# Attention with a top-32 mask and two expert layers on one core: the first five slots written out, the hidden product turned earlier, and the last 64 keys of two heads turned together

## The reference

```python
# attention, for each batch and head
scores = q @ k.T / sqrt(64)
kth    = 32nd largest score of each row
scores = where(scores >= kth, scores, -1e9)
attn   = exp(scores - max);  attn /= attn.sum() + 1e-9
x      = attn @ v                     # heads side by side: 1152 x 512
# gated layer
x2     = ((x @ w_a) * (x @ w_b)) @ w_out      # 512 -> 1536 -> 512
# four experts, weighted by p = probs / sum(probs)
out    = sum over e of p[:, e] * (relu(x2 @ w1[e]) @ w2[e])   # 512 -> 1024 -> 512
```

## Time and profile before

| | us |
|---|---|
| median of 3 runs (lowest to highest) | 847.64 (845.38 to 847.84) |
| the profiled execution, and its span in the trace | 849.11, 847.3 |
| busy: PE, DVE, ACT, POOL | 807.8, 457.9, 384.6, 297.1 |
| chain of work that ended last: PE, ACT, POOL | 88%, 4%, 4% |

### The profile page before, as it was taken

The page is one execution under the profiler, slowest core; times in us unless marked ns, Lnnn a source line. Parts: engine busy times, 40 slices in busy tenths (PEclk is TensorE's granted clock), DMA queues, the critical chain, the costliest instruction groups (busy, mean ns, idle before and its releaser), DMA issues.

```text
span 847.3 us, 13113 instructions
## 1 busy us (share of the span) xinstructions
PE 807.8 (95%) x4985; PEld 713.1 (84%) x4985; DVE 457.9 (54%) x902; ACT 384.6 (45%) x712; POOL 297.1 (35%) x269
## 2 busy tenths in 40 slices
PE   4468999999999999999999999999999999999998
PEld 3346788888888888888889899899899898898996
DVE  5979999899999999998124112122121121221121
ACT  5665787777777777777444011311032010230110
POOL 3766875454545454545331000530016000440000
PEclk9557999999999999999999999999999999999999
DMA  9540685456545654445688500230004100000000
GB/s 233 160 117 1 219 242 206 150 193 200 187 148 183 254 170 158 163 155 173 209 285 300 219 1 1 99 100 1 1 1 141 58 1 1 1 1 38 14 25 38
DMA packets 71631, 102.59 MB, mean 121 GB/s; under 512 B 32528, under 2 KB 48912, under 8 KB 71568
## 3 DMA queue, kind: packets, MB, share of 16 engines
q1 hardware_dynamic: 70512, 101.48, 36.6%
q10 hardware_dynamic: 1056, 0.26, 0.2%
HBM read 88.36 MB, written 13.37 MB: 120 GB/s over the span
## 4 chain that ended last, share of the span: by engine, by line
PE 88%; ACT 4%; POOL 4%; issue 2%; DMA 1%; DVE 1%; SPq 0%; ACTq 0%; POOLq 0%
PE ps L612 24%; PE ps L632 23%; PE ps L522 16%; PE ps L507 8%; PE ps L471 5%; PE ps L442 5%; PE ps L451 4%; PE ps L480 1%; POOL p_sb L1007 1%; ACT p_sb L702 1%; POOL wa_lo L1041 1%; DMA wo<-wo_d 1%; PE ps L402 1%; ACT pT L709 1%; PE ps L514 0%
## 5 line engine op out<-in xcount | busy, mean ns | idle before, releaser
L769 ACT ACTIVATE h_hi<-ps 128x384 fp32r<-128x384 f32 x96 | 47.0, 491 | 269.7 <-PE ps L612 269.5
L874 DVE MAX8 m<-work 128x8 f32<-128x576 f32 x216 | 152.3, 747 | 0.0
L1057 POOL TENSOR_TENSOR w_lo<-w_raw,w_hi 128x2048 fp32r<-128x2048 f32 x12 | 55.1, 4617 | 244.5 <-ACT w_hi L765 244.5
L933 DVE SCALAR_TENSOR_TENSOR h_lo<-ps,h_hi 128x384 fp32r<-128x384 f32 x96 | 53.3, 557 | 156.8 <-ACT h_hi L769 156.8
L612 PE MATMUL ps<-x_hi,w_hi 128*128 128x384 f32 x384 | 129.0, 336 | 0.0
L612 PE MATMUL ps<-x_hi,w_lo 128*128 128x384 f32 x384 | 128.8, 336 | 0.0
L612 PE MATMUL ps<-x_lo,w_hi 128*128 128x384 f32 x384 | 128.8, 335 | 0.0
L632 PE MATMUL ps<-w_hi,h_hi 128*128 128x512 f32 x288 | 112.2, 390 | 0.0
L632 PE MATMUL ps<-w_hi,h_lo 128*128 128x512 f32 x288 | 112.2, 390 | 0.0
L632 PE MATMUL ps<-w_lo,h_hi 128*128 128x512 f32 x288 | 112.1, 389 | 0.0
L880 DVE MATCH_REPLACE8 work<-m,work 128x576 f32<-128x576 f32 x144 | 106.0, 743 | 0.0
(11 more groups left out here) (90 smaller groups left out, 1507.8 us busy)
## 6 DMA issues: line engine op xcount, KB each, us to landing
wo<-wo_d SPq DMA_DIRECT2D x96, 512.0 KB, 4.9
w_raw<-moe_w_in SPq DMA_DIRECT2D x16, 1024.0 KB, 6.6
wo_d<-wo SPq DMA_DIRECT2D x12, 512.0 KB, 4.5
w_raw<-moe_w_a_in SPq DMA_DIRECT2D x4, 768.0 KB, 6.0
w_raw<-moe_w_b_in SPq DMA_DIRECT2D x4, 768.0 KB, 5.5
wo_raw<-moe_w_out_in SPq DMA_DIRECT2D x12, 256.0 KB, 3.9
v_sb<-v_in SPq DMA_DIRECT2D x18, 128.0 KB, 3.8
x_d<-x_hi_out SPq DMA_DIRECT2D x9, 256.0 KB, 3.0
```

The costliest lines, as they stand in the source:

```text
L769: copy(h_hi[:, m, :], ps[:, UP + m % FREE_UP, 0:GN], ACT.Relu).then_inc(ac_r, 1)
L874: nc.vector.max(m8[:, par, i, 8 * r:8 * r + 8], work[:, i, :]).then_inc(ve_top, 1)
L933: nc.vector.scalar_tensor_tensor(h_lo[:, m, :], ps[:, UP + m % FREE_UP, 0:GN], 0.0, h_hi[:, m, :].bitcast(F32), ALU.max, ALU.subtract).the ...
L1057: nc.gpsimd.tensor_tensor(lo[:, s, :], raw[s][:], hi[:, s, :].bitcast(F32), ALU.subtract).then_inc(done, 1)
```

## The change

1. **Last 64 keys.** For the odd head of each pair the keys are stored with the last 64 first. Its 64 last keys then stand next to the 64 last keys of the even head in the probabilities, which now lie in one row without a gap, and one transpose turns both. In v the fifth chunk holds the even heads' rows in partitions 0 to 63 and the odd heads' in 64 to 127, with zeros in the other half for each. Nine transposes for a unit instead of ten; `p_out` copies 512 and 640 columns instead of twice 640. The number of products with v stays. Copying the keys out of PSUM takes two instructions instead of one (for the very first pair the second is done by VectorE). GpSimd zeroes the halves of the second batch's v in slot 12.
2. **First five slots.** TensorE's slots 0 to 4 have an order of their own: the scores of unit n+2 are made in slot n (of n+1 before), after the transposes, and the weighted sum behind them. ScalarE rounds the weight slices behind `p_out` instead of ahead of it (in all slots), and slices 6 and 7 both in slot 4. `scale` and `x_low` of the first tile come after VectorE's steps 1 and 2 of unit 5 instead of 4 and 6.
3. **From slot 5 on.** TensorE does `h_transpose` ahead of `send`. The turning of the inverted sums stands between the transposes of the two heads and writes to another bank. ScalarE does `x_hi` between the two masks, and `y_out` between the two exponentials. VectorE does `sums` after the first MAX8 of a unit instead of the second.

The core of the diff:

```diff
+                first = head * (S + KL)
-                    for c in range(KC):
+                    for c in range(KC - 1):
                         tr = nc.tensor.transpose(ps_pT[head][:, c * P:(c + 1) * P],
-                                                 p_sb[:, head, c * P:(c + 1) * P], ident[:])
+                                                 p_row[:, first + c * P:first + (c + 1) * P], ident[:])
+                    if head:
+                        tr = nc.tensor.transpose(ps_pT[1][:, (KC - 1) * P:KC * P], p_row[:, S - KL:S + KL], ident[:])
...
+            def first_slot(n):
+                if n == 0:
+                    scores(1)
+                else:
+                    p_transpose(n - 1, None)
+                if scaled_tile(n + 1) is not None:
+                    inv_transpose(scaled_tile(n + 1), ps_a)
+                if next_q(n) is not None:
+                    pe.wait_ge(ld_q, 16 + 32 * next_q(n))
+                    q_transpose(range(PR), ps_a)
+                if n < LAG_AB - 1:
+                    scores(n + 2)
+                if n:
+                    weighted_sum(n - 1)
+                if scaled_tile(n + 1) is not None:
+                    pe.wait_ge(po_pick, PR + 1)
+                    inv_spread(scaled_tile(n + 1))
...
                 if n + 1 < NP:
                     scores(n + 1)
+                if u is not None:
+                    h_transpose(u)
                 if sent_of(n) is not None:
                     send(sent_of(n))
-                if u is not None:
-                    h_transpose(u)
...
             def keys_pair(b, pr):
-                copy(kT[:, b, pr, 0:(KC - 1) * P], bank, ACT.Copy).then_inc(ac_k, 1)
+                even = copy(kT[0:D, b, pr, 0:S - KL], bank[0:D, :], ACT.Copy)
+                if (b, pr) == (0, 0):
+                    even.then_inc(ac_k, 1)
+                else:
+                    copy(kT[D:P, b, pr, KL:S], bank[D:P, :], ACT.Copy).then_inc(ac_k, 1)
...
                     below_top(j, 0)
+                if scaled_tile(n) is not None:
+                    x_hi(scaled_tile(n))
+                if j is not None:
                     below_top(j, 1)
...
-            SUMS, SCALE, LOW = 2, 10, 11
-            FIRST_SUMS, FIRST_SCALE, FIRST_LOW = 8, 4, 6
+            SUMS, SCALE, LOW = 1, 10, 11
+            FIRST_SUMS, FIRST_SCALE, FIRST_LOW = 8, 1, 2
```

More of the change, by code:

```diff
@@ L229, in build, with other_half @@
         STEEP = 2.0 ** 96
+        def other_half(b, side):
+            rows = slice((1 - side) * KL, (2 - side) * KL)
+            return v_sb[b][rows, KC - 1, :, :].rearrange("p (r z) d -> p z r d", z=2)[:, side]
         def batch_of(t):
@@ L258, in load_v @@
                     sp.dma_start(v_sb[b][:, 0:KC - 1, h, :], src).then_inc(ld_v[b], 16)
[L259 to L260 removed]
+                for side in range(2):
+                    src = v[b, :, (KC - 1) * P:S, :].rearrange("(r z) s d -> z s r d", z=2)[side]
+                    dst = v_sb[b][side * KL:(side + 1) * KL, KC - 1, :, :].rearrange("p (r z) d -> p z r d", z=2)[:, side]
+                    sp.dma_start(dst, src).then_inc(ld_v[b], 16)
             w1_v = w1.rearrange("e (s k p) f -> e s p k f", s=2, p=P)
@@ L538, in _ @@
                 keys_pair(0, pr)
-            for n in range(LAST + 1):
+            def first_slot(n):
[15 more added lines that the diff above has]
+                    inv_spread(scaled_tile(n + 1))
+            for n in range(LAG_AB):
+                first_slot(n)
+            for n in range(LAG_AB, LAST + 1):
                 m, u = unit_of(n), turned_unit(n)
@@ L668, in keys_tail @@
                 bank = ps[:, 1, first * KL:last * KL] if b else ps_y[:, first * KL:last * KL]
-                copy(kT[:, b, first:last, (KC - 1) * P:S], bank.rearrange("p (r s) -> p r s", s=KL), ACT.Copy).then_inc(ac_k, 1)
+                turned = bank.rearrange("p (r s) -> p r s", s=KL)
+                even = copy(kT[0:D, b, first:last, S - KL:S], turned[0:D], ACT.Copy)
+                if (b, first) == (0, 0):
+                    even.then_inc(ac_k, 1)
+                else:
+                    copy(kT[D:P, b, first:last, 0:KL], turned[D:P], ACT.Copy).then_inc(ac_k, 1)
             def load_first_q(h0, h1, s):
@@ L696, in exponentials @@
                 t, h = n // PR, 2 * (n % PR) + head
-                slot = p_sb[:, head, 0:S]
+                slot = p_sb[:, head, :]
                 act.wait_ge(po_p, 2 * n + head + 1)
@@ L708, in p_out @@
                     act.wait_ge(pe_x, n)
-                    copy(pT[:, head, :, :], ps_pT[head][:, 0:KC * P].rearrange("p (c t) -> p c t", c=KC),
+                    chunks = KC - 1 + head
+                    copy(pT[:, head, 0:chunks, :], ps_pT[head][:, 0:chunks * P].rearrange("p (c t) -> p c t", c=chunks),
                          ACT.Copy).then_inc(ac_pT, 1)
@@ L713, in inv_turned @@
                 act.wait_ge(pe_i, 2 * t + 1)
-                copy(invT[:], ps_a[:, 0:P], ACT.Copy).then_inc(ac_i, 1)
+                copy(invT[:], (ps[:, 3, P:2 * P] if t else ps_a[:, P:2 * P]), ACT.Copy).then_inc(ac_i, 1)
             def inv_out(t):
@@ L788, in _ @@
                     scores_out(n + 1, 0)
-                if scaled_tile(n) is not None:
-                    x_hi(scaled_tile(n))
                 if j is not None:
                     exponentials(j, 0)
+                if finished_tile(n) is not None:
+                    y_out(finished_tile(n))
+                if j is not None:
                     exponentials(j, 1)
@@ L795, in _ @@
                     scores_out(n + 1, 1)
-                if finished_tile(n) is not None:
-                    y_out(finished_tile(n))
                 if u is not None:
@@ L803, in _ @@
                     expert_hi(0, n - NP - 2, 0)
-                for i in HIGH_IN.get(n, ()):
-                    slice_hi(i)
                 for g in CHUNKS_IN.get(n, ()):
@@ L815, in _ @@
                     inv_turned(scaled_tile(n + 1))
+                for i in HIGH_IN.get(n, ()):
+                    slice_hi(i)
                 if finished_tile(n) is not None:
@@ L864, in top_scores @@
                     nc.vector.max(m8[:, par, i, 0:8], s_sb[:, ring[i], :]).then_inc(ve_top, 1)
-                between(n, 2)
+                    between(n, 1 + i)
                 for i in range(2):
@@ L924, in _ @@
             nc.vector.memset(x_inv[:], 0.0).then_inc(ve_z, 1)
-            nc.vector.memset(v_sb[0][KL:P, KC - 1, :, :], 0.0)
-            nc.vector.memset(v_sb[1][KL:P, KC - 1, :, :], 0.0).then_inc(ve_z, 1)
+            for side in range(2):
+                nc.vector.memset(other_half(0, side), 0.0).then_inc(ve_z, 1)
             def low(raw, hi, lo, s, done, ready):
@@ L1036, in _ @@
                     push_down(j, 1)
+                if n == 12:
+                    pool.wait_ge(ac_k, KEYS0 + 1)
+                    pool.wait_ge(po_p, 2 * n)
+                    for side in range(2):
+                        nc.gpsimd.memset(other_half(1, side), 0.0).then_inc(po_z, 1)
+                        pool.wait_ge(po_z, side + 1)
                 for i in LOW_IN.get(n, ()):
```

82 lines of the change are left out of this document (39 added, 43 removed).

## The result

| | before | after |
|---|---|---|
| median of 17 runs each (lowest to highest) | 847.11 (845.38 to 849.32) | 850.20 (847.66 to 851.93) |
| profiled execution, span | 849.11, 847.3 | 850.07, 848.3 |
| busy: PE, DVE, ACT, POOL | 807.8, 457.9, 384.6, 297.1 | 801.5, 459.9, 388.0, 298.4 |

After to before is 1.0033, with an interval of 1.0022 to 1.0044. The kernel has become slower by 3.1 us, where 843.2 and a range of 839.0 to 847.3 were predicted.

What follows compares the result with a forecast made beforehand. TensorE was taken to bound the steady pipeline, something else the first slots. Start 7.3 plus steady slots 4.4 minus last slots 7.3 gave 4.4 us less: 847.64 - 4.4 = 843.2 us, range 839.0 to 847.3.

Steps and rivals of the forecast that it cites:

- The first slots: Start of the kernel: first gated product at 63.2 to 64.6 instead of 71.37; 7.3 us gained, bounds 3.5 and 8.5.
- Rival (a): First slots: xT_lo comes later, GpSimd has begun a slice, the product starts near 67.5; 847 us, chance 0.18.
- Slots 7 to 10: ScalarE's masks wait for GpSimd; the round doesn't get shorter, and fewer transposes and slot 7's new wait vanish in it.
- Steady slots: Slots 11 to 34, with 0.2 us from slots 35 and 36: 4.4 us gained together, bounds 2.5 and 6.5.
- The price of the transpose: Steady slots: one transpose fewer saves 0.10 us a slot, 2.4 us in 24 slots.
- The order without the change of operand type: Steady slots: h transposes ahead of send save 0.05 us a slot, 1.2 us in 24; bounds 0 and 0.09 a slot.
- the 0.6 for `x_hi`: Steady slots: x_hi between the masks makes the low part ready sooner, 6 x 0.1 = 0.6 us gained.
- rival (d): Steady slots: the h transposes wait in each slot and the steady term is lost; 848 us, chance 0.07.
- The last slots: Slots 35 to 40: TensorE waits for h_sb at the h transposes; 7.3 us lost, bounds 5.5 and 8.5.
- the one on the clock: Slots 38 to 40: busy for three quarters with gaps under 3 us, so TensorE's clock was kept at 2.4 GHz.
- Rival (c): Slots 38 to 40: new gaps bring TensorE's clock to 1.2 GHz, adding 15 to 18 us; 859 us, chance 0.05.
- three signs named for a wrong prediction: First gated product later than 67 us, waits for h_sb in steady slots, or last slots no longer than before.

Runs made afterwards that it cites:

- e4: The kernel before with one part of the change alone, the h transposes ahead of send in all slots: 855.74 us, 1.0098 of before.
- e9: e2 with GpSimd's slice in slot 4 held until the sums are inverted, and x_hi of slot 9 behind the first score copy: 838.91 us.
- e1: The changed kernel with send ahead of the h transposes again in all slots: 840.55 us, 0.9918 of before.
- e2: The changed kernel with send ahead of the h transposes from slot 35 on alone: 840.67 us, 0.9921 of before.

## Why the prediction was wrong, by its own steps

The sum was made trace against trace: 4.4 us less. The traces say 1.0 more, so 5.4 us are to be found. The runs say 3.1 more; the other 2 lie in before's profiled execution, which was 2.0 us above the median of its 17 runs (I had 1.5 from three), while after's was 0.1 below its own.

**The first slots: right in kind, and in size with some luck.** Foretold 7.3, found 7.22 between the two traces. The round came out as foretold to 0.3 us, and the product at 64.54, within 63.2 to 64.6. But the five other traces with these first slots have it at 64.89 to 65.96, and e4, whose first slots are those of the kernel before, has it at 70.15 and not 71.37. Over all pairs of these traces the gain in slot 6 is 4.6 to 7.5 us, 6.1 between the means. So the forecast was about 1 us too high here, and the profiled execution of the kernel before, 1.54 us behind e4 in slot 6, hides it. One step was wrong: I had `x_den` free of GpSimd. It lost 2.3 us, which made the scaling later than foretold (61.80, not 60.5). Rival (a), the low part behind a slice, did not happen; a slice did stand in the way, but of the sums.

**Slots 7 to 10: wrong, 1.7 us.** The step "this round doesn't get shorter, and TensorE's fewer transposes and its new wait in slot 7 for the late `h_sb` both vanish in it" priced no loss. About 1.1 us of it is `x_hi` between the masks of slot 9 (e9). I had priced that edit only where it helps, in the steady slots, and not asked what stands behind the waiting instruction in slots in which GpSimd sets the pace. The new waits of the h transposes in slots 7 and 10 (1.34 and 0.55 us) are in the same stretch; behind the first 0.3 us is lost (slots 7 to 8: -7.28, -7.01), behind the second 0.4 (slots 10 to 11). e1, which has `send` first there, loses neither, so the turned order is the rest of it, 0.7 us.

**Steady slots: right for the tile, 0.9 us too much in the sum.** 3.3 us from slot 11 to 34 instead of 4.2. From slot 30 to 34 a tile takes 42.15 us instead of 42.80, as foretold (42.1 and 42.8), but from slot 11 to 18 the lead grows only from 5.52 to 6.22, 0.10 us a slot against 0.16 behind that. One part of what is missing is the second copy of the key pairs, "priced at nothing, at most 0.5 us". I had looked for its price at the masks, but it is the scores that wait: TensorE loses 0.24 us in slot 15 and, ahead of this stretch, 0.34 at the start of slot 11. The price of the transpose held (2.14 measured, with that wait, 2.3 for 23 slots). The order without the change of operand type brings 0.5 to 0.67 us instead of 1.2, so 0.02 to 0.03 us a slot instead of 0.05. The rest, 0.5 to 0.7, fits the 0.6 for `x_hi`; that one was not measured by itself. From 140 to 376 us TensorE waits for `h_sb` in no slot, so rival (d) is out.

**The last slots: waits right, clock wrong, 2.7 us.** The waits were foretold as 1.2, 0.5, 0.1, 1.9, 2.8 and 1.9 us in slots 35 to 40. They are:

```profile
387.74 0.55 PE L495 MATMUL ps<-ident,h_sb 128*128 128x128 f32 x3 [1.09 <-POOL h_sb L1061]
...
397.30 0.55 PE L495 MATMUL ps<-ident,h_sb 128*128 128x128 f32 x3 [0.48 <-POOL h_sb L1061]
...
407.01 0.52 PE L495 MATMUL ps<-ident,h_sb 128*128 128x128 f32 x3
```

and 1.71, 2.99 and 1.71 above. Net, 7.3 was foretold and 7.46 measured. The step that failed is the one on the clock: "Slots 38 to 40 will be busy for three quarters with gaps under 3 us, so they are nearer to the first; I keep 2.4 GHz". The stretch from 10 to 20 us was taken as the measure, busy for half and at 0.97, but the mean over 10 us says nothing on how long its longest gap is. The trace of the kernel before had the answer in the same stretch: TensorE stops at 16.61 us for 11.2 us, and the clock is down 2.8 us later.

```profile
16.60:19.40 2.80, 0.01 (x1) 0.00 (x0) 2.80 (x7) 2.75 (x2) 2.65 (x1) 1.00 1.01 185
19.40:20.00 0.60, 0.00 (x0) 0.00 (x0) 0.60 (x2) 0.00 (x0) 0.60 (x1) 0.52 0.85 195
```

The 0.97 was the start of the fall, not a clock that holds out. In slot 39 one gap of 3.0 us was enough. Rival (c) had this mechanism and the point from which it decides, and was wrong in its size: it supposed that the fall lasts to the end of slot 40 and priced 15 to 18 us, where it came in slot 39, lasted 6.8 us and cost 2.67. With so high a price and a chance of 0.05 it stood outside the sum and the range.

Together 0.1 + 1.7 + 0.9 + 2.7 = 5.4 us, and with 1.6 for where the two profiled executions stand to their medians 843.2 + 5.4 + 1.6 = 850.2. Much of the 1.6 can be the luck of the first slots, since that is where the kernel before is 1.54 us behind e4. No term alone would have left the range; all fell on the same side. None of the three signs named for a wrong prediction came: they watched the first product, the steady slots and the length of the last ones, and not the clock. And the price of the edit that decides was known: 1.2 us foretold for the turned order in the steady slots against 7.3 in the last ones. The prediction held both terms and never set them side by side; e2 does, and keeps the gain.

## What to carry to other kernels

When one line of a pipeline changes for all slots, price its steady slots and its last ones apart and compare the two: an order that is free while other work covers a wait can cost more in a few slots of draining than it gains in thirty. A gap of TensorE can have two prices, its length and what the clock does behind it; here fifteen products of no use in the longest gap took away the second. Before a trace is used to say that the clock will hold, look for its longest gap, and at the clock within it. Where an instruction is put between two others that a second engine waits for (here `x_hi` between two masks), ask in which slots its own input is late.
